# Half-wide token tiles in the first MLP of a gated linear attention with two MLPs, and a new order of its head

## The reference

```python
# attention: B, H, S, D = 4, 8, 768, 48
state = np.zeros((B, H, D, D))
for t in range(S):
    cur = np.einsum('bhd,bhe->bhde', u[None] * kt, vt)
    y[:, :, t] = np.einsum('bhd,bhde->bhe', rt, state + cur)
    state = wt[:, :, :, None] * state + np.einsum('bhd,bhe->bhde', kt, vt)
x = y.transpose(0, 2, 1, 3).reshape(3072, 384)
# first MLP: w_in 384x2048, w_out 2048x384
h = x @ w_in
g = h * np.clip(h + 3.0, 0.0, 6.0) / 6.0
x = g @ w_out
# second MLP: w1, w2 384x1024, w3 1024x1024, w_out2 1024x384
a = x @ w1
b = x @ w2
out = ((a * b) @ w3) @ w_out2
```

## Time and profile before

| | |
|---|---|
| median of 3 runs | 1021.86 us (1020.98 to 1022.7) |
| profiled execution | 1019.5 us, its span 1017.7 us |
| PE, busy share | 93%, 6320 matmul records |
| PE weight loads | 75% |
| DVE | 54% |
| ACT | 30% |
| POOL | 24% |
| mean granted clock | 0.971 |
| DMA | 92.84 MB, mean 91 GB/s |

### The profile page before, as it was taken

One profiled execution on the slowest core, in us unless ns is written; L12 is line 12 of the kernel. 1 busy time (PEld: TensorE's weight loads), 2 busy tenths in 40 slices (PEclk: granted clock), 3 DMA queues, 4 the chain that ended last, 5 costly groups with the idle time before them and its releaser, 6 DMA issues.

```text
span 1017.7 us, 15638 instructions
## 1 busy us (share of the span) xinstructions
PE 944.7 (93%) x6320; PEld 767.6 (75%) x6320; DVE 550.7 (54%) x743; ACT 307.5 (30%) x502; POOL 243.4 (24%) x209
## 2 busy tenths in 40 slices
PE   1579849998999999999999999999999999999998
PEld 1356547786777877777787787787888888888887
DVE  1884558787777677777777752463222222222221
ACT  0113213333333333333333333453213231313122
POOL 0453335344444353435352500000000000000000
PEclk9779959999999999999999999999999999999999
DMA  9953454544342443425333100330101010100000
GB/s 286 293 167 90 137 160 115 142 110 116 110 117 81 114 124 103 127 76 154 86 120 93 62 19 18 118 130 31 62 1 62 1 62 1 62 1 32 1 32 32
DMA packets 79879, 92.84 MB, mean 91 GB/s; under 512 B 9415, under 2 KB 71870, under 8 KB 79678
## 3 DMA queue, kind: packets, MB, share of 16 engines
q1 hardware_dynamic: 69326, 82.13, 27.7%
q10 hardware_dynamic: 10480, 9.70, 3.4%
HBM read 76.07 MB, written 11.01 MB: 86 GB/s over the span
## 4 chain that ended last, share of the span: by engine, by line
PE 77%; DVE 12%; issue 4%; SPq 3%; ACT 2%; DMA 2%; POOL 1%; DVEq 0%; ACTq 0%
PE ps_acc L1023 9%; PE ps_h L1023 8%; PE ps_lv L1051 8%; PE ps_h L1025 8%; PE ps_h L1024 8%; PE ps_acc L1025 8%; PE ps_acc L1024 8%; PE ps_lv L1024 3%; PE ps_lv L1025 3%; PE ps_lv L1023 3%; PE ps_h L1159 3%; DVE k_sb L769 2%; DVE r_sb L769 2%; PE ps_att L1085 2%; SPq L352 2%
## 5 line engine op out<-in xcount | busy, mean ns | idle before, releaser
L569 ACT ACTIVATE g_hi<-gated 128x512 fp32r<-128x512 f32 x144 | 90.9, 632 | 395.1 <-DVE gated L917 261.6
L519 POOL TENSOR_TENSOR tok_a<-tok_a 128x384 f32<-128x384 f32 x120 | 143.2, 1219 | 257.4 <-DMA tok_a<-in_k 257.4
L1051 PEld LDWEIGHTS ps_lv<-r_sb,k_sb 48*128 48x128 f32 (+3 forms) x1792 | 94.3, 179 | 58.5 <-issue 45.1
L1005 DVE TENSOR_TENSOR gated<-gated,ps_lv 128x512 f32<-128x512 f32 x48 | 33.0, 688 | 189.3 <-PE ps_lv L1025 189.3
L1051 PE MATMUL ps_lv<-r_sb,k_sb 48*128 48x64 f32 (+3 forms) x1792 | 101.7, 266 | 35.9 <-DVE A_own L839 22.9
L925 DVE TENSOR_TENSOR g_lo<-gated,g_hi 128x512 fp32r<-128x512 f32 x96 | 79.5, 828 | 88.2 <-ACT g_hi L569 88.2
L1023 PE MATMUL ps_acc<-g_hi,w_out_hi 128*128 128x512 f32 x288 | 122.2, 424 | 0.0
L1023 PE MATMUL ps_h<-x_hi,w_in_hi 128*128 128x512 f32 x288 | 115.4, 401 | 1.9 <-DVE gated L917 1.7
L1024 PE MATMUL ps_h<-x_hi,w_in_lo 128*128 128x512 f32 x288 | 114.8, 399 | 0.0
L1025 PE MATMUL ps_h<-x_lo,w_in_hi 128*128 128x512 f32 x288 | 114.8, 398 | 0.0
L1025 PE MATMUL ps_acc<-g_lo,w_out_hi 128*128 128x512 f32 x288 | 114.4, 397 | 0.0
(11 more groups left out here) (96 smaller groups left out, 1570.0 us busy)
## 6 DMA issues: line engine op xcount, KB each, us to landing
tok_a<-in_r SPq DMA_DIRECT2D x85, 192.0 KB, 3.0
tok_a<-in_w SPq DMA_DIRECT2D x42, 192.0 KB, 3.6
v_sb<-in_v SPq DMA_DIRECT2D x12, 384.0 KB, 3.4
x_scratch<-x_out SPq DMA_DIRECT2D x6, 768.0 KB, 3.8
x_in<-x_scratch SPq DMA_DIRECT2D x6, 768.0 KB, 6.0
tok_a<-in_k SPq DMA_DIRECT2D x22, 192.0 KB, 4.2
w3T_sb<-in_w3T ACTq DMA_DIRECT2D x8, 512.0 KB, 19.6
out<-x_out SPq DMA_DIRECT2D x5, 768.0 KB, 4.0
```

Of the source, the lines that this page charges most:

```text
L519: return nc.gpsimd.tensor_tensor(dst, x, y, ALU.mult)
L569: return nc.scalar.activation(dst, src, ACT.Copy, **scale)
L1005: nc.vector.tensor_tensor(gated[n % 2][:], gated[n % 2][:], ps_lv[:, n % 2, :], ALU.mult).then_inc(ab_made, 1)
L1051: last = nc.tensor.matmul(psum[0:count, h, first:first + C // 2] .rearrange("s (n l) -> s n l", l=size), k_g[rows, cols.start:cols.start + ...
```

## The change

1. A tile of the first MLP is one group of 256 tokens (12 tiles). A slot does two feature blocks, side by side in one bank: `hidden` is 18 matmuls of 256 columns, `project` 18 of 256. There are 12 x 8 = 96 slots as before, and the gate and the splits keep their size of 128x512.
2. `LEAD` is 12: slot 0 has step 4 of group 1. The head has group 0, all of `w34` and four level products of group 1 (three ahead of the first `hidden`, one between the first two).
3. SP's queue starts with w, k and r of group 0, then `w_out2` and `w3T` in two halves; constants go to ACT's queue, and so does half of `move_x` of the first two chunks. Tokens come in three DMAs a chunk instead of seven. k and r have semaphores of their own.
4. DVE makes the token products of chunk 0 only, POOL those of all others. `A_head` is gone: group 1 uses `A_own`. Group 0's levels use `ps_acc` in two pairs of banks, and the bank of y is the fourth of `ps_acc`.
5. Level products leave out rows that no mask keeps (124 and 120 for 128). Weight pieces: nine in the head, seven in slots 0 to 6, one each.
6. The late weights go into slots 86 to 94 (80 to 88 before), and at the end `product(0)` is issued ahead of the last `project`.

```diff
-SLOTS = TILES * NF1
+NP = NF1 // 2
+SLOTS = TILES * NP
...
-LATE_SLOT = (TILES - 1) * NF1
-LEAD = 20
+LATE_SLOT = SLOTS - 1 - LATE
+LEAD = 12
...
-            load_w(0)
-            load_rk(0)
-            load_tok(0)
-            sp.dma_start(u_sb[:], u.to_broadcast([P, DM])).then_inc(consts_loaded, 16)
-            load_tok(1)
...
+            load_w(0)
+            load_k(0)
+            load_r(0)
+            sp.dma_start(w_out2_sb[:], w_out2).then_inc(w_out2_loaded, 16)
+            load_w3T(0)
+            load_tok(1)
+            load_tok(0)
+            load_w3T(1)
+            load_v(0)
             load_w_over(1)
+            load_k(1)
+            load_r(1)
+            for q in range(6):
+                load_weight(q)
             load_tok_over(2)
             load_tok_over(3)
...
             def hidden(n):
-                t, i = divmod(n, NF1)
+                t, i = divmod(n, NP)
                 if i == 0:
-                    pe.wait_ge(x_lo_done, CT * (t + 1))
+                    pe.wait_ge(x_lo_done, 2 * (t + 1))
...
-                for kt in range(KT):
-                    last = three_passes(ps_h[n % 2][:], w_in_hi[:, i, kt, :], w_in_lo[:, i, kt, :],
-                                        x_hi[t % 2][:, kt, :], x_lo[t % 2][:, kt, :],
-                                        kt == 0, kt == KT - 1)
+                for f in range(2):
+                    for kt in range(KT):
+                        last = three_passes(ps_h[n % 2][:, f * GT:(f + 1) * GT],
+                                            w_in_hi[:, 2 * i + f, kt, :], w_in_lo[:, 2 * i + f, kt, :],
+                                            x1_hi[t % 2][:, kt, :], x1_lo[t % 2][:, kt, :],
+                                            kt == 0, kt == KT - 1)
...
             def project(n):
...
                 for d in range(KT):
                     cols = slice(d * P, (d + 1) * P)
-                    last = three_passes(ps_acc[:, d, :], w_out_hi[:, i, cols], w_out_lo[:, i, cols],
-                                        g_hi[n % 2][:], g_lo[n % 2][:], i == 0, i == NF1 - 1)
+                    for f in range(2):
+                        tokens = slice(f * GT, (f + 1) * GT)
+                        last = three_passes(ps_acc[:, d, 0:GT], w_out_hi[:, 2 * i + f, cols],
+                                            w_out_lo[:, 2 * i + f, cols],
+                                            g_hi[n % 2][:, tokens], g_lo[n % 2][:, tokens],
+                                            i == 0 and f == 0, i == NP - 1 and f == 1)
...
-                copy(x2_out[:], ps_acc[:], scale=1.0 / 6.0).then_inc(x2_copied, 1)
+                copy(x2_out[:, :, 0:GT], ps_acc[:, 0:KT, 0:GT], scale=1.0 / 6.0).then_inc(x2_copied, 1)
...
             pe.wait_ge(late_lo_done, LATE)
+            product(0)
+            project(SLOTS - 1)
+            product(1)
             pe.wait_ge(x2_copied, TILES)
-            product(0)
-            for n in range(1, OUT_TILES * NF2):
+            project2(0)
+            for n in range(2, OUT_TILES * NF2):
```

More of the change, by code:

```diff
@@ L376, in move_x @@
                     sp.wait_ge(x_lo_done, g - 1)
-                for head in range(H):
+                for head in range(H // 2 if g < 2 else H):
                     row, at_row = head * D, head % 2 * HB
@@ L555, in _ @@
             start(1)
-            products_by_token(3)
-            start(2)
-            start(3)
-            for p in range(2, GROUPS):
+            for p in range(1, GROUPS):
                 products_by_token(2 * p)
@@ L830, in merge @@
             def merge(p, step):
+                rows = C - (E4 << step)
                 dve.wait_ge(products[p % 2], level(p, step))
@@ L1013, in _ @@
             product(0)
-            for n in range(1, TILES * NF2):
+            for n in range(1, OUT_TILES * NF2):
                 product(n)
-                if n % NF2 == 3 and n // NF2 + 1 < TILES:
+                if n % NF2 == 3 and n // NF2 + 1 < OUT_TILES:
                     split_x2(n // NF2 + 1)
```

459 lines of the change are left out of this document (215 added, 244 removed).

## The result

The changed kernel took 988.83 us (median of 4 runs, 987.18 to 991.18) beside 1022.28 for the kernel before: ratio 0.9678, 95% interval 0.965 to 0.9706. It is faster, as forecast, and inside the range; the forecast of 978 us was 10.8 us too low. The profiled execution took 987.18 us with a span of 985.4, to be set against a sum of 974.7.

What follows compares the result with a forecast made beforehand. A head of 150 us set by waits, then 867 us of almost pure PE work. Span 1017.7 - 60 + 15 + 2 = 974.7; 1.8 us around the span and 2.4 to the median gave 978 us, range 961 to 1001.

Steps and rivals of the forecast that it cites:

- B: Rival: in the first MLP each 256-column matmul pays a handover that wider ones hide; 48 us more, 1026; chance 0.05.
- C: Rival: weight loads of the first MLP not hidden at all at 256 columns; 380 us more, about 1358; chance 0.02.
- D: Rival: head gains little; GpSimd's chunks, token loads and low clock push first `hidden` to about 112; 1000 us; chance 0.06.
- A: Rival: in the first MLP the weight load limits each 256-column matmul to 0.121 us; 993 us; chance 0.12.
- Part 1: Start of the head: group 0's loads alone in front bring the first level product near 11 us instead of 20.54.
- Part 3: Head: READ_B of group 0 waits for `update(0)`, behind chunk 3's band sum on DVE; 5 us idle (0 to 8).
- Part 2: PE's work in the head: `w34` about 44 us, eleven attention steps 21 us, low clock 9 us.
- Part 5: First MLP: two matmuls of 256 columns take as long as one of 512, 0.1167 us each; 0 us.
- Part 6: 256-token tiles: `x2_tile` copy hidden; 2 us wait for `x_lo` before `product(0)` gives back what the order wins; 0 us.
- Part 4: Slots: 84 attention steps instead of 76 give 15 us back, plus 2 us of added slot waits.
- second cold opening (+3): Head: 3 us for another low-clock opening on PE, within the 9 us of low clock.
- row-group rule: Skill's rule: loads overlap matmuls only where the row group differs, so all 3456 first-MLP matmuls would pay their load.

## Why the prediction was right, and where it was off

The shape was right: a head cut by 56 us (150.34 to 93.93), some 14 us back in the slots, matmuls of 256 columns that hide their loads, no wait at a tile's end, and a second MLP that takes the time it took. Rivals B and C fell with the pace (0.1183; B decided from 0.129), D with a first `hidden` far from 112, and A, which needed 0.121, came about a third true.

The 10.7 us between the sum (974.7) and the span (985.4) come from these steps:

| step | forecast | measured | us |
|---|---|---|---|
| Part 1, first level product | 11 | 15.04 | +4.0 |
| Part 3, waits of PE in the head behind it | 5 | 10.3 (7.78, 1.67, 0.84) | +5.3 |
| Part 2, PE's work in the head, with low clock | 74 | 68.6 | -5.4 |
| Part 5, 3456 matmuls of 256 columns | 0.1167 | 0.1183 | +5.7 |
| Part 6, wait ahead of `product(0)` | 2 | 4.17 | +2.2 |
| Part 6, low clock behind that wait | none | 12 matmuls 0.43 apart | +2.4 |
| Part 4 and the rest, as remainder | | | -3.5 |

- **Part 1** failed on the term "4 to 5 us of transfer after about 2 of latency": first `scale` at 10.92 for 7.5. The run with group 0 ahead of `w_out2` shows the landing near 10 us whatever stands behind it, and the rings busy at 203 to 227 GB/s, where the term took 285, with 1.70 MB to move and not 1.34: the constants on ScalarE's queue were left out. The 285 was a mean over 60 us; its four slices from 6 to 12 us read 226 to 283. The other 0.5 us of the row is DVE's, 0.42 of it a wait for `r_sb` at 12.63.
- **Part 2** was sound. `w34` takes 46.3 us with one cold opening of 2.6, so 43.7 without it (44 forecast). Low clock cost 7.7 us in this profile (9 forecast; each row at it less the same row at the high one), and 3.9 more in the second profile of the same code; the forecast's "second cold opening (+3)" lies between the two kinds (1.9 and 5.8 us). The eleven steps took 17 us, not 21: 1.89 us a step was a remainder of the slots and holds more than the steps' own work.
- **Part 3** held in its mechanism: the wait, its place, its releaser, the landing of chunk 2 (52.45, forecast 50 to 55) and the chain, since GpSimd runs from 52.45 to 70.33 without a gap. Two things were missing. PE's waits of 1.67 and 0.84 us at two level products had no term, and with the 7.78 for 5 they make the row. And the landing of chunk 3's tokens was not priced: it lies near 59.5, 1.1 us ahead of GpSimd's being free, so the chain alone decides by no more than that, and that both limits give nearly the same time is luck.
- **Part 4** held: 12.7 us of idle in the slots ahead of the last wait, where the forecast has 15.3 less the 1.59 of the old last wait, 13.7. DVE ends each of them, the longest 3.48 us.
- **Part 5** was taken "because 384 columns with the same loads are nearest". The halves alone show the step to 256 by itself: 0.2333 for one of 512, 0.2366 for two of 256. The Trainium skill (TensorE: Matmul & The Clock Gate, Back-to-back issue gap) gives, for the gap of an isolated matmul, a constant of 2.5 ns beside the columns, by which I worked out an estimated 4 us and then set it aside. Here the pair costs 3.3 ns more than the single one, so on this step trace and rule nearly agree, and my sentence that the trace disagrees was wrong for 256 columns. The 384 columns, at 0.1733, lie under the 0.1758 midway between 256 and 512, so one constant doesn't give all three. The row-group rule that I weighed there stays refuted: the loads are hidden.
- **Part 6** failed on the place of `x_lo`: I took it over from the kernel before (711.05, 2 us behind PE) and overlooked that on DVE a late weight, a gate and a `g_lo` now stand ahead of it, 670.40 to 673.6, and that ACT's `x_hi` waits for the same gate. PE stood 4.17 us, and the low clock behind it cost 2.4 more, for which there was no term. "What it wins is given back" became a loss; the last `project` first is about 4 us better.

**What stays open:** why 256 columns take 1.6 ns more than half of 512. Two loads in a row can start 0.11 us apart, less than 0.1183, but a limit by the load and a fixed cost of each matmul are both possible, and no run separates them. Nor is it shown what decides whether the clock comes back at 77 or at 85 in one and the same program, the chip among the candidates, or why the DMA engines move 213 GB/s in the first loads and 390 later.

## What to carry to other kernels

A wait of 4 to 10 us on TensorE cost its length and then 3.4 to 12.6 us at the low clock behind it, and how long it stayed low differed between two profiles of the same code. To end the wait 2 us earlier is a gain that such a scatter hides; independent matmuls put into it gave one that is clear of it, together with the last `project` first (0.9622 against 0.9685 for the last `project` first alone). When an operation is moved past another across a boundary, list what stands ahead of its operand on the engine that makes it, not only how long that operand takes. And take the same program's profile twice before believing a difference of a few us, or compare only profiles in which the clock came back alike.
